# Turning the attention probabilities in 64-row halves, with the PSUM banks of the transposes divided anew

## The reference

```
scores = q @ k.T / 8 + bias[h]         # bias: a small MLP of log-distances, by head
attn   = exp(scores - rowmax); attn /= rowsum + 1e-9
x      = attn @ v                       # as (2304 tokens, 512)
h      = max(x @ w1, x @ w2, x @ w3) ; x = h @ w_out            # 512 -> 768 -> 512
h      = x @ w_in ; g = 0 below -1, h above 1, (h+1)^2/4 between
out    = g @ w_out2                                             # 512 -> 2048 -> 512
```

## Time and profile before

| what | value |
|---|---|
| median of three runs | 1107.71 us |
| the profiled execution's own time | 1108.04 us |
| its span, first to last instruction | 1106.3 us |
| TensorE matmul busy | 1048.8 us (95%) |
| VectorE busy | 557.0 us (50%) |
| ScalarE busy | 510.1 us (46%) |
| GpSimd busy | 313.1 us (28%) |
| all transposes of the probabilities (L956) | 640 matmuls, 93.3 us busy |
| mean granted clock of TensorE | 0.993 of full speed |

### The profile page before, as it was taken

One profiled execution on the slowest core, in us unless ns is written; L12 is line 12 of the kernel. 1 busy time (PEld: TensorE's weight loads), 2 busy tenths in 40 slices (PEclk: granted clock), 3 DMA queues, 4 the chain that ended last, 5 costly groups with the idle time before them and its releaser, 6 DMA issues.

```text
span 1106.3 us, 18896 instructions
## 1 busy us (share of the span) xinstructions
PE 1048.8 (95%) x6648; PEld 921.8 (83%) x6648; DVE 557.0 (50%) x1313; ACT 510.1 (46%) x1082; POOL 313.1 (28%) x544
## 2 busy tenths in 40 slices
PE   5869999999999889999999999999999999999997
PEld 2348777777777679999999999999998999989996
DVE  8948667766667522322223222675444454444543
ACT  7958666666667443221212122554344343443432
POOL 5028667766767456000000023560000000000000
PEclk9989999999999999999999999999999999999999
DMA  3561241332421134000000011221001010010101
GB/s 129 206 210 44 51 143 34 87 108 51 122 59 42 50 95 133 1 1 0 0 0 0 0 39 57 88 84 29 1 1 28 0 29 0 0 28 0 29 1 29
DMA packets 80798, 55.61 MB, mean 50 GB/s; under 512 B 44896, under 2 KB 66400, under 8 KB 80736
## 3 DMA queue, kind: packets, MB, share of 16 engines
q1 hardware_dynamic: 80736, 54.82, 17.1%
HBM read 39.46 MB, written 15.34 MB: 50 GB/s over the span
## 4 chain that ended last, share of the span: by engine, by line
PE 78%; DVE 8%; issue 6%; DMA 2%; SPq 2%; ACT 2%; POOL 1%; DVEq 1%; ACTq 0%
PE ps L1000 38%; PE ps L1044 18%; PE ps L1012 7%; PE ps L926 4%; PE ps L956 4%; PE ps L944 4%; DVE s_sb L752 3%; DVE xT L715 2%; DMA bias_h<-bias_scratch 2%; DVE k_lo L770 2%; PE ps L911 1%; DVE pt_t L761 1%; ACT probs L577 1%; DVEq L715 1%; SPq L288 1%
## 5 line engine op out<-in xcount | busy, mean ns | idle before, releaser
L1000 PE MATMUL ps<-x_hi,w_hi 128*128 128x384 f32 x816 | 274.6, 336 | 3.8 <-DVE x_lo L792 3.5
L1000 PE MATMUL ps<-x_hi,w_lo 128*128 128x384 f32 x816 | 274.4, 336 | 0.0
L1000 PE MATMUL ps<-x_lo,w_hi 128*128 128x384 f32 x816 | 273.8, 336 | 0.0
L752 DVE CUSTOM_DVE_ANT_0 s_sb<-ps,bias_h 128x576 f32<-128x576 f32 (+1 forms) x160 | 120.1, 752 | 84.5 <-issue 60.5
L502 POOL TENSOR_TENSOR w_lo<-raw,w_hi 128x256 fp32r<-128x256 f32 x108 | 83.5, 805 | 277.4 <-ACT w_hi L611 277.4
L1000 PEld LDWEIGHTS ps<-x_hi,w_hi 128*128 128x128 f32 x816 | 153.8, 188 | 9.1 <-issue 4.0
L1000 PEld LDWEIGHTS ps<-x_lo,w_hi 128*128 128x128 f32 x816 | 153.7, 188 | 3.9
L1000 PEld LDWEIGHTS ps<-x_hi,w_lo 128*128 128x128 f32 x816 | 153.6, 188 | 0.0
L577 ACT ACTIVATE probs<-s_sb,row_min 128x576 f32<-128x576 f32 (+1 forms) x160 | 124.7, 779 | 40.9 <-DVE row_min L752 40.8
L461 POOL TENSOR_SCALAR probs<-probs,row_inv 128x512 f32<-128x512 f32 (+1 forms) x160 | 108.7, 693 | 90.4 <-DVE row_inv L732 88.7
L1044 PE MATMUL ps<-w_hi,g_lo 128*128 128x512 f32 x288 | 113.9, 395 | 0.0
(11 more groups left out here) (95 smaller groups left out, 1662.6 us busy)
## 6 DMA issues: line engine op xcount, KB each, us to landing
bias_scratch<-probs SPq DMA_DIRECT2D x36, 288.0 KB, 2.1
bias_h<-bias_scratch SPq DMA_DIRECT2D x7, 1152.0 KB, 6.6
raw<-in_moe_w_out SPq DMA_DIRECT2D x22, 256.0 KB, 3.1
raw<-in_moe_w SPq DMA_DIRECT2D x18, 256.0 KB, 3.0
out<-o_sb SPq DMA_DIRECT2D x36, 128.0 KB, 2.4
q_in<-in_q SPq DMA_DIRECT2D x32, 128.0 KB, 2.3
k_in<-in_k SPq DMA_DIRECT2D x32, 128.0 KB, 2.4
v_in<-in_v SPq DMA_DIRECT2D x32, 128.0 KB, 2.3
```

Source lines behind the costliest of these rows:

```text
L752: dve.tensor_tensor_reduce(halves(s_sb[0:n, (par + t) % 2, :]), score_ps(m, t)[0:n], halves(bias_h[0:n, par, t, :]), 1.0, 3.0e38, ALU.add, ...
L1000: last = pe.matmul(ps[:, bank, 0:BLK], w[:, at:at + P], x[:, kt, :], start=(kt == 0 and n == 0), stop=(kt == KT - 1 and n == 2))
```

## The change

The four full probability tiles are transposed in twos: tiles 0 and 1 as `p01` at t = 1, tiles 2 and 3 as `p23` at t = 3. Each 128x128 block is transposed as two halves of 64 rows, from partitions 0 to 63 and 64 to 127; the first half's result goes to bank 5 and the second's to bank 6. ScalarE copies both tiles of p01, VectorE both of p23, each with two instructions that read both banks. A two waits for the copies of the two before it. The other transposes (q, k, qk, p4, tail) all use bank 7, and each waits for the consumer of the one before it. The slots are now in the order q; p01, k; qk; p23; p4; tail.

```diff
--- before.py
+++ after.py
@@ -197,8 +197,9 @@
 
         STEPS = range(-1, PAIRS + 3)
         Q_AT, K_AT, QK_AT = 0, 1, 2
-        BY_ACT = ("p0", "p2", "q", "k", "qk")
-        BY_DVE = ("p1", "p3", "p4", "tail", "k", "qk")
+        BY_ACT = ("p01", "q", "k", "qk")
+        BY_DVE = ("p23", "p4", "tail", "k", "qk")
+        P_NAME = {1: "p01", 3: "p23", 4: "p4"}
 
         def has(m, lag):
 
@@ -207,8 +208,8 @@
         def names_of(m):
 
             for t in range(NT):
-                if has(m, 1):
-                    yield f"p{t}"
+                if has(m, 1) and t in P_NAME:
+                    yield P_NAME[t]
                 if has(m, -1) and t in (Q_AT, K_AT, QK_AT):
                     yield {Q_AT: "q", K_AT: "k", QK_AT: "qk"}[t]
             if m % 2 == 0 and has(m, 2):
@@ -218,11 +219,21 @@
         SLOT = {at: n for n, at in enumerate(SLOTS)}
         ACT_COUNT = {at: sum(x[1] in BY_ACT for x in SLOTS[:n + 1]) for n, at in enumerate(SLOTS)}
         DVE_COUNT = {at: sum(x[1] in BY_DVE for x in SLOTS[:n + 1]) for n, at in enumerate(SLOTS)}
-        T_BANKS = 3
-
-        def t_bank(m, name):
-
-            return 5 + SLOT[m, name] % T_BANKS
+        TWOS = ("p01", "p23")
+        TWO_SLOTS = [at for at in SLOTS if at[1] in TWOS]
+        ONE_SLOTS = [at for at in SLOTS if at[1] not in TWOS]
+        ONE_BANK = 7
+
+        def two_ps(t):
+
+            at = t % 2 * 2 * P
+            return ps[:, 5:7, at:at + 2 * P]
+
+        def held_by(m, name):
+
+            slots = TWO_SLOTS if name in TWOS else ONE_SLOTS
+            n = slots.index((m, name))
+            return slots[n - 1] if n else None
 
         rows = [P] * T + [HALF]
         PART_A, PART_B = range(0, 3), range(3, NT)
@@ -552,7 +563,7 @@
                 def turned(name):
 
                     act.wait_ge(t_ps, SLOT[m, name] + 1)
-                    return ps[:, t_bank(m, name), :]
+                    return ps[:, ONE_BANK, :]
 
                 def output(i, half):
 
@@ -563,12 +574,13 @@
 
                 for t in range(NT):
                     n = rows[t]
-                    if has(m, 1) and f"p{t}" in BY_ACT:
-
-                        src = turned(f"p{t}")
-                        act.activation(p_t[:, (m - 1) // 2 % 2, e, :, t * P:t * P + n],
-                                       src[:, 0:T * n].rearrange("p (c n) -> p c n", c=T),
-                                       ACT.Copy).then_inc(t_act, 1)
+                    if has(m, 1) and t == 1:
+                        act.wait_ge(t_ps, SLOT[m, "p01"] + 1)
+                        for x in (0, 1):
+                            last = act.activation(p_t[:, (m - 1) // 2 % 2, e, :, x * P:(x + 1) * P]
+                                                  .rearrange("p c (r j) -> p r c j", r=2),
+                                                  two_ps(x).rearrange("p r (c j) -> p r c j", c=T), ACT.Copy)
+                        last.then_inc(t_act, 1)
                     if has(m, 0):
                         act.wait_ge(s_bias, NT * m + t + 1)
                         if m >= 2 and t == 0:
@@ -756,7 +768,7 @@
 
                     if t == 0 and par == 1 and has(m, 3):
                         i = (m - 3) // 2
-                        copy_tail = ps[:, t_bank(m - 1, "tail"), 0:MAIN]
+                        copy_tail = ps[:, ONE_BANK, 0:MAIN]
                         dve.wait_ge(t_ps, SLOT[m - 1, "tail"] + 1)
                         dve.tensor_copy(pt_t[:, i % 2, 0:MAIN], copy_tail).then_inc(t_dve, 1)
                     if t == 0 and has(m, 1):
@@ -767,17 +779,24 @@
 
                         if t == K_AT + 1:
                             dve.wait_ge(t_act, ACT_COUNT[m, "k"])
-                            dve.tensor_tensor(k_lo[:, e, 0:MAIN], ps[:, t_bank(m, "k"), 0:MAIN],
+                            dve.tensor_tensor(k_lo[:, e, 0:MAIN], ps[:, ONE_BANK, 0:MAIN],
                                               k_hi[:, e, 0:MAIN].bitcast(F32), ALU.subtract).then_inc(t_dve, 1)
                         if t == QK_AT + 1:
                             dve.wait_ge(t_act, ACT_COUNT[m, "qk"])
-                            dve.tensor_tensor(k_lo[:, e, MAIN:S], ps[:, t_bank(m, "qk"), P:P + HALF],
+                            dve.tensor_tensor(k_lo[:, e, MAIN:S], ps[:, ONE_BANK, P:P + HALF],
                                               k_hi[:, e, MAIN:S].bitcast(F32), ALU.subtract).then_inc(t_dve, 1)
-                    if has(m, 1) and f"p{t}" in BY_DVE:
-                        src = ps[:, t_bank(m, f"p{t}"), :]
+                    if has(m, 1) and t >= 3:
+                        src = ps[:, ONE_BANK, :]
                         i = (m - 1) // 2
-                        last = copy(f"p{t}", p_t[:, i % 2, e, :, t * P:t * P + n],
-                                    src[:, 0:T * n].rearrange("p (c n) -> p c n", c=T))
+                        if t == 3:
+                            dve.wait_ge(t_ps, SLOT[m, "p23"] + 1)
+                            for x in (2, 3):
+                                last = dve.tensor_copy(p_t[:, i % 2, e, :, x * P:(x + 1) * P]
+                                                       .rearrange("p c (r j) -> p r c j", r=2),
+                                                       two_ps(x).rearrange("p r (c j) -> p r c j", c=T))
+                        else:
+                            last = copy("p4", p_t[:, i % 2, e, :, t * P:t * P + n],
+                                        src[:, 0:T * n].rearrange("p (c n) -> p c n", c=T))
                         if t == T and par == 0:
                             last = dve.tensor_copy(pt_t[:, i % 2, MAIN:S], src[:, T * n:NT * n])
                         last.then_inc(t_dve, 1)
@@ -895,14 +914,24 @@
 
                 def open_slot(name):
 
-                    n = SLOT[m, name]
-                    if n >= T_BANKS:
-                        held = SLOTS[n - T_BANKS]
-                        if held[1] in BY_DVE:
-                            pe.wait_ge(t_dve, DVE_COUNT[held])
-                        else:
-                            pe.wait_ge(t_act, ACT_COUNT[held])
-                    return t_bank(m, name)
+                    held = held_by(m, name)
+                    if held is not None and held[1] in BY_DVE:
+                        pe.wait_ge(t_dve, DVE_COUNT[held])
+                    elif held is not None:
+                        pe.wait_ge(t_act, ACT_COUNT[held])
+                    return ONE_BANK
+
+                def turn_two(t0):
+
+                    pe.wait_ge(p_norm, NT * (m - 1) + t0 + 2)
+                    open_slot(P_NAME[t0 + 1])
+                    for t in (t0, t0 + 1):
+                        for c in range(T):
+                            for r in range(2):
+                                half = slice(r * HALF, (r + 1) * HALF)
+                                last = pe.transpose(two_ps(t)[:, r, c * HALF:(c + 1) * HALF],
+                                                    probs[half, e, t, c * P:(c + 1) * P], ident[half, half])
+                    last.then_inc(t_ps, 1)
 
                 def turn_rows(name, x):
 
@@ -917,7 +946,7 @@
                     cols = O_COLS[half]
                     if half == 0:
                         pe.wait_ge(vv_in[i % 2], 64 * (i // 2 + 1))
-                        pe.wait_ge(t_act, ACT_COUNT[2 * i + 2, "p2"])
+                        pe.wait_ge(t_act, ACT_COUNT[2 * i + 2, "p01"])
                         pe.wait_ge(t_dve, DVE_COUNT[2 * i + 2, "tail"])
                     if 2 * i + half >= 1:
                         pe.wait_ge(o_ok, 2 * i + half)
@@ -945,12 +974,14 @@
                                                  kx[:, par, c * HC:(c + 1) * HC],
                                                  start=(part == 0), stop=(part == 1))
                         last.then_inc(s_ps, 1)
-                    if has(m, 1):
+                    if has(m, 1) and t in (1, 3):
+                        turn_two(t - 1)
+                    if has(m, 1) and t == T:
                         n = rows[t]
                         pe.wait_ge(p_norm, NT * (m - 1) + t + 1)
                         if t == T and par == 0:
                             pe.wait_ge(tail_norm, NT * m)
-                        bank = open_slot(f"p{t}")
+                        bank = open_slot("p4")
                         pr = probs[0:n, e, t, :]
                         for c in range(T):
                             last = pe.transpose(ps[:, bank, c * n:(c + 1) * n], pr[:, c * P:(c + 1) * P],
```

## The result

The changed kernel takes 1216.26 us (median of 4, 1215.69 to 1219.34) against 1107.65; the ratio is 1.099 (95% interval 1.097 to 1.101). The forecast of 1212 us is met, but its sum was wrong in two places that nearly cancelled. The profiled execution has a span of 1215.0 us, 108.7 more than the 1106.3 of before.

What follows compares the result with a forecast made beforehand. TensorE bounds the attention (busy 94 us of 100). Waits at the single bank 7 add 14 x 7.08 = 99.1 us in step pairs, other steps 2.8, 2.4 and some 3, bias -3: +104, 1108.04 becomes 1212 us; range 1186 to 1255.

Steps and rivals of the forecast that it cites:

- q waits for the tail behind B0: Odd step: q waits for VectorE's tail copy behind B0, starting at 2.41 us instead of 0.51; 14 times of 1.9.
- qk waits for k_lo behind p01's copies and E1: Before qk, TensorE idles 2.1 us in even and 2.4 us in odd steps, as k_hi stands behind ScalarE's earlier work.
- k waits for q_s in even steps: Even step: k waits for q_s, which stands behind E0, until 3.23 us; the idle time around p01 hides its price.
- Sixteen halves at 0.06 us each, 0.98: TensorE's 64-row transposes of p01 or p23: sixteen take 0.98 us, at the pace of p4's row.
- The fast end of the bound (0.49): If two halves pass at once, sixteen take 0.49 us, 0.43 less a two than before the change.
- 0.21 us at each change of shape: TensorE's loads stand still 0.21 us going in and out of p01 and p23; ends 0 and 0.49 each.
- The forecast's steps of 12.82 and 13.66 us: Lengths forecast for the changed attention's steps: even 12.82 us (+2.78), odd 13.66 us (+4.30).
- Two banks in one copy, priced at nothing: Copies reading both banks cost nothing extra; on the path twice a step (p01), a tenth more would be 3 us.
- The clock, at 12 chances in 100: Rival: idle times lower TensorE's clock to 1.2 GHz; 1377 us for the whole attention, 1250 for a quarter; 12 in 100.
- the forecast's lower end of 1190: With fast halves and no drains, steps grow by 2.40 (even) and 3.23 us (odd): +82, 1190 us.
- The prediction's test ("if the steps lengthen though the clock is low"): Sign in the trace after the change that the forecast is wrong; the other was a wait before qk under 1 us.

Runs made afterwards that it cites:

- k_hi first: Changed kernel, but ScalarE writes k_hi directly behind E1 and copies p01 after it: 1175.32 us, 1.062.
- tail first: Changed kernel, but VectorE copies the tail out of bank 7 before B0 of the odd step: 1197.45 us, 1.081.
- both orders: Changed kernel with VectorE copying the tail ahead of B0 and ScalarE writing k_hi ahead of p01's copies: 1172.93 us, 1.058.
- whole tiles: Changed kernel with its slots, but each tile transposed in whole 128x128 blocks into one bank of its own, 5 or 6: 1194.80 us, 1.078.
- the three with the wait filled: Eight idle score matmuls before qk's wait, added to the changed kernel (1183.34 us), to it with both reorderings (1154.28), to it with whole 128x128 transposes (1185.21).

## Why the prediction was right, and where it was not

- *q waits for the tail behind B0*: right in place, number and size (2.42 us into the step, 14 times).
- *qk waits for k_lo behind p01's copies and E1*: right in place and in its 30 times; the loads stood still 2.1 us on average (63.7 / 30). That it hangs on ScalarE's order alone was too simple: with k_hi first, the steps got shorter by 0.28 and 0.56 us only, and VectorE's B2 was next.
- *k waits for q_s in even steps*: right, 15 times.
- *Sixteen halves at 0.06 us each, 0.98*: the mis-sized term. They take 0.57 us of loads, 0.65 up to the next group: by turns of rows and banks they pass in about half the time that p4's have in one row group and one bank. The fast end of the bound (0.49) was nearer than the value taken. (At its own 0.06 the row gives 0.96, not 0.98.)
- *0.21 us at each change of shape*: 0.16 in front of the halves, none behind them. The forecast's steps of 12.82 and 13.66 us were 12.04 and 12.37 at full clock, some 29 us too many over the 14 pairs. The halves' pace is on the path three times a pair (3 x 0.33 us, 14 us in all), the gaps are 0.6 us a pair (8 us). The rest is shorter latencies, such as p01's, which could be copied 0.11 us after the next group's first load (213.46 to 213.57) and not 0.31.
- *Two banks in one copy, priced at nothing*: right, p01's two copies take 1.07 to 1.09 us where the forecast's prices give 1.11 (0.52 + 0.59).
- *The clock, at 12 chances in 100 and priced at 1250 us if it fell for a quarter of the attention*: this rival came true beside the forecast, in part. At a mean clock of 0.88 the low level held for about a quarter of the attention, and it cost 33 to 35 us, where that price had some 40. The argument against it, that TensorE is never nearly idle for 4 us in a steady step, was true as a fact (no pause was longer than 2.3 us) and did not keep the clock up: it fell behind pauses of 0.7 and 1.8 us with a little work between them (the step at 170.12). The step at 197.24 has the same pauses and kept its clock, so they do not settle it by themselves.
- The two errors cancel: 70 + 35 us in the attention and 3 elsewhere were measured, where 104 us of waits alone were forecast. That the number came so near is luck: the waits alone would have given about 1181 us (1108 + 70 + 3), below the forecast's lower end of 1190 and below its range from 1186. The prediction's test ("if the steps lengthen though the clock is low") could not tell a wait from a low clock; the step lengths at full clock did.
- The Trainium skill (TensorE: Matmul & The Clock Gate, Part 3) says that a weight load overlaps running matmuls only if its row group differs. The halves' pace of (0.57 - 0.14) / 15 = 0.03 us from start to start, with p4's 0.06 beside it, agrees; but rows and banks alternate together here, and no run separates them.
- The Trainium skill (TensorEngine Tiling (Array Packing), Key Properties) says that a change of tiling mode drains TensorE. The 0.16 and 0.39 us in front of changed shapes agree, but no gap stood behind the halves.

## What to carry to other kernels

Before resources are regrouped, write down for each slot who releases the previous one and what stands ahead of that release on its engine: here a faster transpose was paid for with three such waits, while another bank for one slot and a new order of two other engines' work gave, with the same halves, a kernel 1.2% faster than the one before. When TensorE gets pauses, compare steps of equal work at both clocks before you explain their length; a chain that only waits and a clock that falls look alike in the total. A few idle matmuls in a pause that cannot be avoided are a quick test, and can be a gain over the same kernel without them.

## What the runs showed of the hardware that was not expected

- TensorE's clock went to its low level (1.2 GHz) for parts of most steps, though no pause was longer than 2.3 us, and rose again in the busy stretch behind it. A step at a mean clock of 0.86 to 0.88 is 1.3 to 1.6 us longer than one at full clock, the few at 0.76 to 0.78 are 2.6 to 3.0 longer. Filling 1.0 us of a 2.1 us pause held the clock at 2.4 GHz and made the kernel 33 us faster.
- The longest pause does not tell how often it falls. Of the 27 steps m = 4 to 30 so many had a low clock for a part; beside them stands the longest idle time of the matmuls in these steps:

| version | steps with a low clock | longest idle time, us |
|---|---|---|
| changed kernel | 21 | 2.03 |
| tail first | 20 | 1.77 |
| k_hi first | 1 | 1.65 |
| both orders | 14 | 1.46 |
| whole tiles | 6 | 2.18 |
| the three with the wait filled | 0 | 1.65, 0.73, 1.65 |

What decides this stays open, and with it whether the filled wait helps by its shorter pause or by its work.
- The sixteen halves, by turns of two row groups and two banks, start 0.03 us apart on average, halves of one row group in one bank 0.06, whole blocks 0.11 to 0.12.
